# Splitting K ahead of the norm on VectorE in the attention stage of a three-stage Trainium2 kernel

## The reference

```python
scores = scale * np.matmul(q, k.transpose(0, 1, 3, 2))      # B=4, H=8, S=768, D=64
is_global = pos[None, :] < n_global                         # 8
is_local = (rel >= 0) & (rel < n_local)                     # 96
keep = is_global | is_local
scores = np.where(keep, scores + bias, -1000000000.0)
scores = scores - np.max(scores, axis=-1, keepdims=True)
a = np.exp(scores)
a = a / (np.sum(a, axis=-1, keepdims=True) + 1e-09)
out = np.matmul(a, v)
```

## Time and profile before

| | |
|---|---|
| three runs | 808.23, 809.03, 809.03 us (median 809.03) |
| the profiled execution | 809.03 us, of which its span is 807.3 us |
| granted TensorE clock, mean over the span | 0.975 |
| TensorE matmuls | 752.7 us busy, 93% |
| VectorE | 536.9 us, 67% |
| ScalarE | 453.4 us, 56% |
| attention stage | 0 to about 216 us |
| both expert layers | from about 220 us to the end |

### The profile page before, as it was taken

The page is one execution under the profiler, slowest core; times in us unless marked ns, Lnnn a source line. Parts: engine busy times, 40 slices in busy tenths (PEclk is TensorE's granted clock), DMA queues, the critical chain, the costliest instruction groups (busy, mean ns, idle before and its releaser), DMA issues. The chain is left out here.

```text
span 807.3 us, 15740 instructions
## 1 busy us (share of the span) xinstructions
PE 752.7 (93%) x5588; PEld 676.4 (84%) x5590; DVE 536.9 (67%) x1463; ACT 453.4 (56%) x919; POOL 165.3 (20%) x184
## 2 busy tenths in 40 slices
PE   2899999999869999999999929999999999999997
PEld 2899999999738998899988816888888888888895
DVE  6877878778388768775566557666676767675420
ACT  3899999989425545465454304555545454636360
POOL 8100000000030322213221101141414142323221
PEclk9999999999979999999999957999999999999999
DMA  8999989986265457634663007868676777769861
GB/s 180 218 214 251 227 195 251 217 227 177 107 180 196 156 216 250 217 129 165 228 233 122 18 2 248 201 198 202 204 188 209 186 220 187 220 180 303 225 126 44
DMA packets 64106, 151.65 MB, mean 188 GB/s; under 512 B 12294, under 2 KB 15750, under 8 KB 64016
## 3 DMA queue, kind: packets, MB, share of 16 engines
q1 hardware_dynamic: 52512, 114.77, 48.6%
q0 software_dynamic: 11504, 35.72, 18.3%
HBM read 118.84 MB, written 16.67 MB: 168 GB/s over the span
## 5 line engine op out<-in xcount | busy, mean ns | idle before, releaser
L1817 PE MATMUL r_ph<-r_xh,r_w1h 128*128 128x384 f32 x256 | 90.7, 354 | 0.0
L1817 PE MATMUL r_ph<-r_xh,r_w1l 128*128 128x384 f32 x256 | 86.2, 337 | 0.0
L1817 PE MATMUL r_ph<-r_xl,r_w1h 128*128 128x384 f32 x256 | 85.8, 335 | 0.0
L592 ACT ACTIVATE pr<-pr,nmx 128x232 f32<-128x232 f32 (+1 forms) x192 | 79.9, 467 | 4.1 <-DVE nmx L685 2.6
L1098 PE MATMUL m_ph<-m_xh,m_w1h 128*128 128x224 f32 x288 | 81.0, 281 | 0.1
L1252 ACT ACTIVATE m_hh<-m_ph 128x224 fp32r<-128x224 f32 (+1 forms) x72 | 25.1, 349 | 98.0 <-PE m_ph L1098 94.1
L1098 PE MATMUL m_ph<-m_xh,m_w1l 128*128 128x224 f32 x288 | 79.1, 275 | 0.0
L1098 PE MATMUL m_ph<-m_xl,m_w1h 128*128 128x224 f32 x288 | 79.0, 274 | 0.0
L685 DVE CUSTOM_DVE_ANT_0 pr<-sc,bias 128x232 f32<-128x232 f32 (+1 forms) x192 | 65.1, 375 | 19.4 <-PE sc L466 16.4
L599 ACT ACTIVATE prt<-tp 128x384 f32<-128x384 f32 (+1 forms) x128 | 65.3, 535 | 20.4 <-PE tp L478 17.0
L1831 PE MATMUL r_py<-r_w2h,r_hh 128*128 128x512 f32 x192 | 76.1, 397 | 0.0
(11 more groups left out here) (298 smaller groups left out, 1960.7 us busy)
## 6 DMA issues: line engine op xcount, KB each, us to landing
r_w<-moe_w SPq DMA_DIRECT2D x64, 512.0 KB, 5.1
m_w<-moe_w SPq DMA_DIRECT2D x36, 512.0 KB, 5.6
row_buf<-moe_w SPq DMA_DIRECT2D x9, 2048.0 KB, 8.7
r_w2l<-r_w POOLq DMA_DIRECT2D x32, 512.0 KB, 4.9
k_raw<-kI SPq DMA_DIRECT2D x64, 208.0 KB, 7.2
q_raw<-qT SPq DMA_DIRECT2D x64, 192.0 KB, 8.2
vo<-vL SPq DMA_DIRECT2D x16, 384.0 KB
x_rows<-row_buf SPq DMA_DIRECT2D x4, 1536.0 KB, 6.6
```

What stands on the lines that cost most here:

```text
L592: nc.scalar.activation(pr[n % PRS][:, t, lo:CW], pr[n % PRS][:, t, lo:CW], ACT.Exp, bias=nmx[n % PRS][:, t:t + 1], scale=-1.0).then_inc(ex ...
L1817: last = nc.tensor.matmul(ph[m % 4][:, 0:CAP], w[:, c, m * P:(m + 1) * P], x[:, c, :], start=(c == 0 and a == 0), stop=(c == KC - 1 and a ...
```

## The change

In VectorE's loop the part of a split that falls into a step now stands ahead of the norm that falls into the same step, where it stood behind it. Both depend only on things that other engines make, and not on each other.

```diff
                         if 1 <= n < H:
                             biases(n)
+                        g, c = n // 6 + 1, n % 6 - 2
+                        if g < PAIRS and 0 <= c < PARTS:
+                            split(g, c)
                         for hd in range(HEADS):
                             if norm_step(hd) == n:
                                 norm(nlink, hd)
-                        g, c = n // 6 + 1, n % 6 - 2
-                        if g < PAIRS and 0 <= c < PARTS:
-                            split(g, c)
```

## The result

| | before | changed |
|---|---|---|
| median of the runs | 808.64 us (808.23 to 809.03) | 813.43 us (812.87 to 814.51) |
| ratio to before | 1 | 1.0066, 95% interval 1.0053 to 1.0080 |
| the same in a second comparison | 808.51 us | 813.51 us, ratio 1.0054 (1.0037 to 1.0071) |
| profiled execution, its span | 809.03, 807.3 us | 815.21, 813.5 us |

The forecast was 814.5 us, in a range of 812.7 to 816.8. The medians of four runs each differ by 4.8 us, the ratio says 5.3. In all, twelve runs of the changed kernel are on record, from 812.87 to 815.21 us, with a median of 814.3.

What follows compares the result with a forecast made beforehand. The prediction took TensorE to set the pace of the attention stage. A cost of 0.39 us at each of 14 places gave 5.5 us, which added to 809.03 us made 814.5 us, range 812.7 to 816.8.

Steps and rivals of the forecast that it cites:

- What bounds: Attention stage: TensorE is busiest and hardly waits; VectorE's late results cost what exceeds TensorE's slack, each excess in full.
- Steps 1 to 3: At 14 places VectorE's split waits 0.4 us for ScalarE's copy, the norm ends 1.51 later, TensorE's L489 load 0.51 late.
- Step 4: Next maxima and ScalarE's copies 0.35 us late, beside TensorE's 0.51: 0.39 a place; 0.46 by the skill page's first statement.
- the meeting: TensorE's next turned unit, 113.62 us at n = 46: TensorE arrives 114.01, ScalarE's release 113.97; the later counts, 0.39 us.
- The sum: 14 places in the attention stage at 0.39 us each: 5.5 us on top of 809.03 us.
- the first place: First of the 14, n = 10: slack 0.77 us, could cost up to 0.75, counted at 0.39 like the others.
- What was to cost nothing: K's low half earlier, part 3's loads 0.35 us later, three later stores some 1.5 us; stages behind keep their lengths.
- Not slower: ScalarE's copy is done in time, the norm 1.05 us late, exactly its slack: 0.00 to 0.01 us a place; 5%.
- The delays did not add up: Rival: ScalarE's late copies also wait for TensorE's late load, 0.86 us a place, 12.0 in all, 821.1 us; 4%.
- TensorE's clock did not fall: Rival: each stall leaves one TensorE step at 1.2 instead of 2.4 GHz, 28 us in all, 837.4 us; 1%.

Runs made afterwards that it cites:

- older rows: Against the changed kernel, turn_gate reads the rows of the pair of heads before, so TensorE's wait for the late norm goes: 811.95 us, ratio 1.0041.
- faster order: Against the kernel before, part 2 of the split moved behind the next step's maxima: 807.73 us, ratio 0.9981; second comparison 807.85 us, 0.9986.
- half copy: Against the changed kernel, ScalarE's copy of K for part 2 of pairs 2 to 15 cut to half its columns: 809.82 us, ratio 1.0015.
- seven places: Against the changed kernel, the split stands ahead of the norm for even pairs only, 7 of the 14 places: 811.79 us, ratio 1.0029.
- older rows, old order: Against the kernel before, turn_gate reads the rows of the pair of heads before, VectorE's order unchanged: 807.07 us, ratio 0.9980.
- half subtraction: Against the changed kernel, VectorE's subtraction L661 for part 2 of pairs 2 to 15 cut to half its columns: 807.83 us, ratio 0.9994.

## Why the prediction was right, point by point

**What bounds.** TensorE sets the pace of the stage. In the changed kernel it is no longer busy throughout. Windows of 42 to 200 us (busy time of TensorE's matmuls, its weight loads, VectorE, ScalarE and GpSimd, then clock, DMA share, GB/s), before and changed:

```profile
42.00:200.00 158.00, 158.00 (x1393) 157.05 (x1393) 122.70 (x439) 144.21 (x310) 0.00 (x0) 1.00 0.94 218
42.00:200.00 158.00, 154.83 (x1353) 151.99 (x1352) 118.12 (x426) 139.64 (x300) 0.00 (x0) 1.00 0.90 209
```

TensorE lost 158.00 − 154.83 = 3.2 us of matmul time there, and the weight loads 157.05 − 151.99 = 5.1.

**Steps 1 to 3** came out to within 0.02 us: 14 waits; the split 0.03 us behind the copy after 0.38 us of idling (0.4 forecast); the load 0.05 us behind the norm's end, standing 0.50 (0.51 forecast); L661 with 19.3 us in 29 waits (19 in 29 forecast).

**Step 4** was the one with two answers. The maxima start at 115.17, 0.08 us before L700's end at 115.25, as at 31.38 in the earlier trace rows. For this pair of instructions that goes against the first statement of the Trainium skill, page "VectorE: DVE Perf Modes", section "The DRAIN you can't avoid", that the next operation waits for an empty pipeline; the same section has an operation that is not held start earlier, and the trace shows such an earlier start. The delays meet where I put them, and a place costs 12.66 − 12.27 = 0.39 us, as forecast. But the way to this 0.39 was in part luck. Compare TensorE's weight loads before (first group) and changed (second): the turned unit before the meeting, the one at the meeting, and the rows turned behind it:

```profile
111.47 0.36 PEld L478 LDWEIGHTS tp<-ident,pr 128*128 128x128 f32 x3
113.62 0.42 PEld L478 LDWEIGHTS tp<-ident,pr 128*128 128x128 f32 x4
114.00 0.36 PEld L489 LDWEIGHTS tp<-ident,row_buf 128*128 128x128 f32 x3
...
114.45 0.35 PEld L478 LDWEIGHTS tp<-ident,pr 128*128 128x128 f32 x3
116.96 0.46 PEld L478 LDWEIGHTS tp<-ident,pr 128*128 128x128 f32 x4
117.39 0.36 PEld L489 LDWEIGHTS tp<-ident,row_buf 128*128 128x128 f32 x3
```

From the turned unit before to the one at the meeting it is 2.15 us before (111.47 to 113.62) and 2.51 changed (114.45 to 116.96), 0.36 more; with the late norm taken away (older rows) it is 2.51 too. So at the meeting the two delays are equal to within 0.01 us, and it can't be said that TensorE's is the later one: the load stands 1.36 us behind the exps in the changed kernel (115.60 to 116.96), as it does with the older rows (114.51 to 115.87), where it waits for them. I had TensorE arrive the whole 0.51 late. It stood 0.50, but reached the score load 1.52 us behind L489 (115.30 to 116.82) in place of 1.57 (111.79 to 113.36), so 0.05 came back. The same 0.05 is lost again behind the meeting: the rows follow the turned unit after 0.43 us (116.96 to 117.39) where TensorE did not stand, and after 0.38 where it did (113.62 to 114.00, and 115.87 to 116.25 with the older rows). That makes the 0.04 us between 0.39 and the 0.35 of the maxima's delay alone. Why TensorE is quicker behind a wait was not tried.

**The sum** gave 5.5 us. The trace of the changed kernel has 5.1 in the stage. The last norm's weight load stands at 223.06 against 216.95, 6.1 us later, of which 14.27 − 13.30 = 0.97 lie before the first matmul:

```profile
14.27 0.55 PE L465 MATMUL sc<-kk,qh 128*128 128x256 f32 x1 [14.27 <-POOL alive L432]
```

The term that was off is the first place, which I counted at 0.39 like the others. Its meeting, before and changed:

```profile
40.01 0.42 PEld L478 LDWEIGHTS tp<-ident,pr 128*128 128x128 f32 x4 [0.39 <-issue]
...
41.00 0.46 PEld L478 LDWEIGHTS tp<-ident,pr 128*128 128x128 f32 x4
```

The distance from the first place to the second was 12.54 us before, not 12.27, because TensorE stood 0.39 us there anyway in place of 0.12 (the prediction has such a wait and used it only to stay at 0.39 in place of 0.75), and is 12.66 now, so it grew by 0.12 where the others grew by 0.39. That 0.27 us of old waiting took up most of the first place's delay: it costs about 0.1 us, an estimate from these distances, and the other 13 cost 0.39 each, 5.2 us in all. The rest of the 1.1 us between the forecast and the median of 813.43 is the starting point, 809.03, which lies 0.4 above the median of four, and the scatter of the runs.

The 0.97 us are no effect of the change. They lie ahead of n = 10, where the queues first differ; in two executions of the same faster order, on two chips, the first matmul stands at 13.37 and at 14.39; and among the runs with the changed order there are 13.22 and 14.37. What sets it was not tried. From the first matmul to the load of the first place it is 24.57 and 23.71 us in those two executions, so single traces tell the start of the stage only to about 1 us. What is firm of the 5.1 is the steady part: from the load of the second place to that of the last it is 147.21 us before and 151.90 changed, 4.7 more.

**What was to cost nothing** did. From the last norm's load to the end of the span it is 590.4 us before (216.95 to 807.3) and 590.4 changed (223.06 to 813.5), so the shift was handed on whole. That they agree so closely is in part chance: over all twelve traces this stretch takes 588.2 to 590.8 us, and not by the order of VectorE: it is 589.4 in the second trace of the changed kernel. The loads behind the later store brought no new row to the list of waits.

**The rivals.** Not slower: the half copy shows it where its condition is made true, at 0.04 us a place and not the 0.00 to 0.01 forecast, since the norm is then 1.16 us late and not 1.05. The delays did not add up; they lie side by side. TensorE's clock did not fall at the places: it is 1.00 from 31 to 217 us through 14 waits at L489, and score loads stay 0.12 us apart. But it did fall once in the stage, ahead of the first place, in both traces of the changed kernel and in that of the half copy. Three microseconds, before and changed, and TensorE's waits ahead of them in the changed kernel:

```profile
27.50:30.50 3.00, 3.00 (x28) 2.96 (x27) 3.00 (x15) 2.67 (x8) 0.00 (x0) 1.00 1.03 228
27.50:30.50 3.00, 3.00 (x16) 3.00 (x16) 3.00 (x14) 2.33 (x6) 0.00 (x0) 0.50 1.03 227
...
21.09 0.68 PE L506 MATMUL op<-vo,prt 128*128 128x128 f32 x4 [1.25 <-ACT prt L599]
26.73 0.49 PE L506 MATMUL op<-vo,prt 128*128 128x128 f32 x2 [1.89 <-ACT prt L599]
```

A granted clock of 0.50 is the lower level, 1.2 GHz; TensorE got through 16 matmuls there in place of 28. The queues do not differ yet at this point, and the same order ran without the fall in other traces (seven places, older rows), so it is no effect of the change. What it cost in these executions can't be told from the scatter at the start of the stage. So the 1.41 us of the earlier trace rows, after which the clock stayed, did not show that every gap of this order leaves it alone. That the waits of 0.5 us at the places do is shown by the places themselves. The Trainium skill, page "TensorE: Matmul & The Clock Gate", section "What's actually happening", says that activity lifts the throttled state; the trace agrees in that the clock was back at 1.00 from 31 us on, with TensorE busy all of 27 to 31 us.

## What to carry to other kernels

Ahead of an instruction that other engines wait for, do not put one that itself waits; an engine far from its limit can still set the time through the order of its queue. Ask for each result how long before its reader it is ready: with 1.05 us of slack, and 0.12 us of standing further on, a norm 1.07 us later cost nothing (the half subtraction), one 1.16 later 0.04 us (the half copy), and one 1.5 later, with the maxima late beside it, 0.39. When an edit makes two results late, look for the place where both delays meet before adding or choosing: there the later one counts, and removing one alone can buy next to nothing (0.04 of 0.39 us here, with the late norm removed).

## What the runs showed of the hardware

A half-size instruction did not take half the time. ScalarE's copy of 832 columns took 0.89 us and that of 416 took 0.54, VectorE's subtraction 1.02 and 0.59. The first matmul of the same kernel stood at 13.37 us in one execution and at 14.39 in another on another chip, against a spread of 3.2 us in its runs (805.82 to 809.00 us); over the twelve traces it stood at 13.15 to 13.37 five times and at 14.16 to 14.55 seven times. TensorE's granted clock fell to 0.50 behind waits of 1.25 and 1.89 us (changed kernel) and behind one of 1.77 (half copy). It stayed at 1.00 behind one of 1.41 (before), behind 1.25 and 1.69 (older rows, old order), and through waits of 0.5 and of 1.14 us, one for each pair of heads. Behind a wait TensorE made up 0.05 us (1.52 us from L489 to the score load in place of 1.57). Distances inside the trace repeated to 0.02 us around their mean while the run times scattered by 3 us; for effects below 0.2% they are the better yardstick.
